# Linear-attention and mixture kernel on one core: order of the products' squares, places of the last chunk, and a weight load in three earlier quarters

## Chip, cores and metric

One core of one Trainium2 chip (trn2). The metric is the device time of one execution in microseconds; a change is told against the median of the runs of the kernel before, 618.05 us (617.24 to 618.30, 3 runs).

## What is computed

Inputs are q, k, v, a_re and a_im of 4 batches, 8 heads, 768 steps and 48 channels. The reference, cut to what matters:

```python
mag = sqrt(a_re**2 + a_im**2); scale = minimum(mag, 0.999) / (mag + 1e-6)
for t in range(768):                       # a complex decaying state for each head, 48 x 48
    S_re, S_im = ar*S_re - ai*S_im + k[t] v[t]^T, ar*S_im + ai*S_re
    y[t] = q[t] @ S_re
x = y as [3072, 384]
logits = x @ phi                           # 32 slots: 8 experts x 4
slot_in = softmax(logits, axis=tokens).T @ x
slot_out[e] = relu(slot_in[e] @ w1[e]) @ w2[e]      # w1[e] 384x1024, w2[e] 1024x384
x = softmax(logits, axis=slots) @ slot_out
out = relu(x @ w_in)**2 @ w_out            # 384 -> 2048 -> 384
```

## The kernel before, in words

Every engine has one program, written out by hand, and they meet only at semaphores. The recurrence is worked in 24 chunks (NT) of 128 steps, six (NC) to each of four batches (B). A batch p needs a **preparation** before its chunks: ScalarE (ACT) and VectorE (DVE) form the magnitudes of a in three tiles t (squares `take_squares`, sum `norm2`, logarithm and exponential `log_m2`, `magnitude`, `log_mag`, reciprocal `inv_mag`, L401, and the cut at 0.999 `bend`, L406); DVE multiplies (`normalise`, L767, three instructions); ACT makes the signed planes (`sign_planes`, L441, nine short copies). Then DVE runs the **chain of products** (`one`, L930): `init_products` (L777), 15 `product_step`s, three `block_step`s, the sum of squares of the first three quarters `square_sums(p, 0)` (L829, 128x1728), the turn factors (L835) and the last quarter's sum `square_sums(p, 1)` (128x576). The squares for these sums come from ACT (`product_squares`, L412: part 0 waits for the second-last block step, part 1 for the last). ACT takes the logarithm of the sums (`all_log_sums`, L428, two loads of the activation table around it), exponentials of it for the first chunk and then for the other five (`exponential`, L435).

The loops of DVE (L969) and ACT (L538) go over p and the chunk c: beside the chunks of batch p - 1 (n = 6(p - 1) + c) they prepare batch p (the chain) and batch p + 1 (the magnitudes). In this text "boundary p" is the place where loop p ends and loop p + 1 begins; boundaries 0, 1 and 2 are the ones with p < B - 1. On DVE a chunk is `key_query` (L878) twice with `weigh` (L870) between, `build_turn` (L896), and two masks `apply_mask` (L908) of the chunk before; steps of the chain stand between them as the shares of `parts` (L926) and `go` (L952) say. At c = 5 the order is: chunk's own work, chain up to the last block step, first sum of squares (for p > 0), the two masks, turn factors, second sum of squares; then the next p begins with the three `normalise`, `key_query`, `weigh` (which waits for the first exponential), `key_query`, `build_turn`, `init_products` (which waits for all signed planes).

On ACT at c = 4 the order is: three `inv_mag`, three `bend` (L555), then the chunk's copies of PE's results (`exponentials` of the softmax, `copy_kt` twice), the first squares (L591), `copy_y`, `copy_state`, the second squares, `copy_sums`, `copy_x`, `copy_raw`; at c = 5 `all_log_sums`, the first exponential, the signed planes, the other exponential, and only then `copy_y`.

TensorE (PE) does for each chunk `scores` (L1115, waits for the stacked inputs, which SyncE's DMAs bring over from DVE's output), `outputs` (L1152), `next_state` (L1131), a transpose of x (`turn_x`, L1188) and the `logits` (L1174); for every pair of chunks `flip` (L1199, transposes of the exponentials) and `weighted_sums` (L1210). `keep_busy` (L1110) fills gaps with idle matmuls. y has PSUM bank 5, x bank 6, the logits and the state share bank 4, scores use banks 0 to 3, the sums bank 7. Behind the last chunk come the slots' experts (PE L1287, L1309) and the last two products, from about 392 us on, which are half of the kernel's time.

The expert weights (16 tiles of 1.5 MB, two halves each from ACT's queue at the chunks' starts in loops 3 and 4, the others from SyncE's) go where the recurrence's tiles lie, as these come free. `EARLY` names six tiles that lie on the start of `big`. Three quarters of tile 6 lie on its columns 4 PF to 5 PF, which the recurrence never uses, and the last quarter on `N_` (5 PF), which the chain does use.

Of the kernel before, what the change touches and what calls it, by code (L numbers as in the profile page):

```python
# [42 lines left out]
def program(nc, a_all, xq_all, v_all, phi, w1, w2, w_in, w_out, out):  # L43
    with ExitStack() as ctx:
# [120 lines left out]
        def sk_ps(half, off, cols):  # L165
# [11 lines left out]
        et_ps = [ps[:, 6, NU * XR:NU * XR + 2 * SL]] * (NT - 1) + [ps[:, 4, 0:2 * SL]]  # L177
        sums_ps = ps[0:SR, 7, 0:DX]

# [6 lines left out]
        log_ready, inv_ready, bent, own_bent, an_ready = (sem("log_ready"), sem("inv_ready"), sem("bent"), sem("own_bent"),  # L186
                                                          sem("an_ready"))
# [6 lines left out]
        y_copied, x_done, x_copied = sem("y_copied"), sem("x_done"), sem("x_copied")  # L194
        lgt_done, raw_copied, max_ready = sem("lgt_done"), sem("raw_copied"), sem("max_ready")
# [32 lines left out]
        LOADED = [48 if k == 5 else 32 if k in EARLY + [10] else 16 for k in range(2 * NX)]  # L228
# [129 lines left out]
        def _(act):  # L358
# [82 lines left out]
            def sign_planes(b, t):  # L441
                act.wait_ge(an_ready, DT * b + t + 1)
# [23 lines left out]
            def copy_y(m):  # L466
                act.wait_ge(y_done, m + 1)
                if m >= 2:
                    act.wait_ge(x_done, m - 1)
                nc.scalar.activation(xts[:, m % 2], y_ps, ACT.Copy).then_inc(y_copied, 1)  # L470

            def copy_raw(m):
# [4 lines left out]
                nc.scalar.activation(eb[0:SR, j % 2, m % 2 * CH:(m % 2 + 1) * CH], lgt_ps, ACT.Copy, scale=-1.0).then_inc(raw_copied, 1)  # L477
# [60 lines left out]
            for p in range(B + 1):  # L538
                for c in range(NC + 2 * (p == B)):
                    n = (p - 1) * NC + c  # L540
                    if p == B - 1:
# [4 lines left out]
                    if p < B - 1:  # L546
# [7 lines left out]
                        elif c == 4:  # L554
                            for t in range(DT):  # L555
                                inv_mag(p + 1, t)
                            for t in range(DT):
                                bend(p + 1, t)
# [12 lines left out]
                    if p == B and c < NC:  # L571
# [3 lines left out]
                        load_half(NC + c)  # L575
# [15 lines left out]
                    if p < B and c == NC - 2:  # L591

                        product_squares(p, int(p == B - 1), 0)
                        product_squares(p, int(p == B - 1), 1)
# [15 lines left out]
                    if p < B - 1:  # L610
# [5 lines left out]
                        elif c == 4:  # L616
                            product_squares(p, 1, 0)
                            product_squares(p, 1, 1)
                    if pair is not None:
# [5 lines left out]
                    if n == NT:  # L625
                        copy_raw(n - 1)
# [841 lines left out]
```

## Time and profile before

| | |
|---|---|
| runs of the kernel before | 618.05 us median, 617.24 to 618.30 |
| the profiled execution | 617.78 us, span 616.1 us, mean granted clock of TensorE 0.934 |
| busy over the span | PE 512.4, DVE 392.4, ACT 339.4, POOL 138.4 us |
| up to about 60 us | DVE alone: magnitudes and the chain of batch 0 |
| 60 to 283 us | loops 1 to 3: chunks 0 to 17 beside the chains |
| 283 to 356 us | loop 4: chunks 18 to 23 |
| 356 to 392 us | experts |
| from 392 us | last products, PE busy throughout |

The views give, for one profiled execution, start and duration of instructions in microseconds from the span's first one; in brackets stands how long the engine had been idle and what ended that.

### The profile page before, as it was taken

The numbers are of one execution on the slowest core, as the hardware profiler recorded it, in microseconds if no ns is written. First come the engines' busy times: TensorE is split into PE (matmuls) and PEld (weight loads), VectorE is DVE, ScalarE is ACT, GpSimd is POOL, SyncE is SP. The second block draws the span as 40 slices with busy tenths as digits, with TensorE's granted clock in tenths as the row PEclk, the third lists the DMA queues.
The fourth block names the chain that finished last, engine by engine and source line by source line (L and its number), as shares of the span: only waits on it lengthen the run. The fifth ranks groups of instructions, "written<-read, shape, count | busy, mean of one in ns | idle before, by whom it ended". The sixth has DMA issues, their size and how long they took to land.

```text
span 616.1 us, 11719 instructions
## 1 busy us (share of the span) xinstructions
PE 512.4 (83%) x4566; PEld 386.4 (63%) x4566; DVE 392.4 (64%) x649; ACT 339.4 (55%) x593; POOL 138.4 (22%) x118
## 2 busy tenths in 40 slices
PE   1000459995998869997999999999999999999997
PEld 1000147774667646775788644578888888888886
DVE  5899999979999799995353151599423333233322
ACT  6818714697456953375243412676655555555653
POOL 7000000000000000000000000266555555555553
PEclk9655589997999979997999999999999999999999
DMA  7400575647655358886799999200101001010101
GB/s 272 153 1 0 113 207 129 146 93 193 170 119 147 71 152 205 231 210 145 190 278 257 422 426 421 99 1 2 53 0 53 0 1 51 2 51 2 53 0 52
DMA packets 41319, 79.59 MB, mean 129 GB/s; under 512 B 7344, under 2 KB 28976, under 8 KB 40112
## 3 DMA queue, kind: packets, MB, share of 16 engines
q1 hardware_dynamic: 39104, 67.44, 38.3%
q10 hardware_dynamic: 2160, 11.40, 5.3%
q8 instruction: 36, 0.59, 0.4%
q14 instruction: 19, 0.16, 0.1%
HBM read 55.12 MB, written 4.72 MB: 97 GB/s over the span
## 4 chain that ended last, share of the span: by engine, by line
PE 61%; DVE 24%; ACT 5%; issue 5%; DMA 3%; SPq 2%; DVEq 0%; ACTq 0%
PE ps L1397 10%; PE ps L1393 10%; PE ps L1394 10%; PE ps L1127 7%; PE ps L1113 4%; DVE tt L798 4%; PE ps L1367 3%; DVE big L772 3%; DVE tt L800 3%; DVE big L804 3%; PE ps L1184 2%; PE ps L1170 2%; DMA stk<-xout 2%; PE ps L1167 2%; PE ps L1287 2%
## 5 line engine op out<-in xcount | busy, mean ns | idle before, releaser
L1092 DVE TENSOR_TENSOR qs<-rs 128x512 f32<-128x512 f32 x96 | 82.7, 861 | 118.8 <-ACT rs L674 118.8
L735 POOL TENSOR_TENSOR hlo<-qs,hhi 128x512 fp32r<-128x512 f32 x96 | 126.1, 1313 | 125.0 <-DVE qs L1092 119.8
L1113 PE MATMUL ps<-ident 128*32 128x512 bf16 x274 | 81.3, 408 | 52.7 <-DVE xout L894 52.7
L1393 PE MATMUL ps<-hhi,who 128*128 128x512 f32 x285 | 110.9, 389 | 0.0
L1394 PE MATMUL ps<-hhi,wlo 128*128 128x512 f32 x285 | 110.9, 389 | 0.0
L674 ACT ACTIVATE rs<-ps 128x512 f32<-128x512 f32 x96 | 57.4, 598 | 82.2 <-PE ps L1367 82.1
L1127 PE MATMUL ps<-stk 112*128 112x224 f32 (+1 forms) x384 | 77.8, 358 | 12.7 <-DMA stk<-xout 12.7
L1127 PEld LDWEIGHTS ps<-stk 112*128 112x128 f32 x384 | 69.5, 199 | 23.9 <-DMA stk<-xout 18.3
L1397 PE MATMUL ps<-hlo,who 128*128 128x512 f32 x285 | 80.5, 391 | 0.1
L727 POOL MEMSET sinz<- 128x768 f32 x1 | 0.7, 738 | 335.9 <-PE ps L1170 335.9
L1113 PEld LDWEIGHTS ps<-ident 128*32 128x32 bf16 x274 | 23.0, 100 | 77.7 <-DVE xout L894 53.0
L678 ACT ACTIVATE hhi<-rs 128x512 fp32r<-128x512 f32 x96 | 60.8, 633 | 3.1
L1397 PEld LDWEIGHTS ps<-hlo,who 128*128 128x128 f32 x285 | 53.2, 188 | 12.2 <-POOL hlo L735 1.3
L1393 PEld LDWEIGHTS ps<-hhi,who 128*128 128x128 f32 x285 | 53.5, 188 | 11.2
L1394 PEld LDWEIGHTS ps<-hhi,wlo 128*128 128x128 f32 x285 | 53.5, 188 | 11.1
L915 DVE TENSOR_TENSOR asb<-ps,mask 128x512 f32<-128x512 f32 x48 | 32.5, 686 | 28.7 <-ACT kts L458 14.5
L458 ACT ACTIVATE kts<-ps 128x384 f32<-128x384 f32 x40 | 19.5, 487 | 52.4 <-PE ps L1127 52.4
L894 DVE TENSOR_TENSOR xout<-big,xq 128x768 f32<-128x768 f32 x48 | 45.7, 953 | 0.5
L1367 PE MATMUL ps<-cst,ust 128*128 128x512 f32 x96 | 37.4, 392 | 0.2 <-DVE ust L1074 0.2
L1170 PE MATMUL ps<-asb,vr 128*48 128x128 f32 x384 | 35.5, 273 | 0.0
L1167 PE MATMUL ps<-stk,st 112*48 112x128 f32 x320 | 31.8, 276 | 0.0
L1184 PE MATMUL ps<-xts,phs 112*32 112x128 f32 x576 | 28.3, 294 | 3.4 <-issue 2.9
(152 smaller groups left out, 795.5 us busy)
## 6 DMA issues: line engine op xcount, KB each, us to landing
stk<-xout SPq DMA_DIRECT2D x144, 128.0 KB, 3.7
wt<-in_w SPq DMA_DIRECT2D x8, 1536.0 KB, 15.2
wt<-in_w ACTq DMA_DIRECT2D x14, 768.0 KB, 6.1
big<-in_a_all SPq DMA_DIRECT2D x12, 768.0 KB, 5.5
xq<-in_xq SPq DMA_DIRECT2D x24, 384.0 KB, 4.2
vr<-in_v_all SPq DMA_DIRECT2D x24, 192.0 KB, 4.1
out<-ost SPq DMA_DIRECT2D x5, 768.0 KB, 3.5
wins<-in_w_in SPq DMA_DIRECT2D x1, 3072.0 KB, 19.8
```

The source lines that it names most:

```text
L674: nc.scalar.activation(rs[:, i % NQS, :], ps[:, i % 2, :], ACT.Relu).then_inc(relu_ready, 1)
L678: nc.scalar.activation(hhi[:, i % NHS, :], rs[:, i % NQS, :], ACT.Square).then_inc(hi_ready, 1)
L735: pool.tensor_tensor(hlo[:, i % NHS, :], qs[:, i % NQS, :], hhi[:, i % NHS, :].bitcast(F32), ALU.subtract).then_inc(lo_ready, 1)
L894: dve.tensor_tensor(o, e, x, ALU.mult).then_inc(kq_ready, 1)
L1092: dve.tensor_tensor(qs[:, i % NQS, :], rs[:, i % NQS, :], rs[:, i % NQS, :], ALU.mult).then_inc(sq_ready, 1)
L1113: nc.tensor.matmul(ps[P - SL:P, bank, :], idb[:, 0:SL], idle, start=True, stop=True)
L1127: last = nc.tensor.matmul(ps[:, h // 2, h % 2 * SK:h % 2 * SK + cols], x[:, 0:CH], x[:, CH:CH + cols], start=True, stop=True)
L1170: last = nc.tensor.matmul(y, vr[:, n % NV, h * D:(h + 1) * D], asb[:, n % 2, h], start=(c == 0), stop=True)
L1367: nc.tensor.matmul(ps[:, i % 2, :], ust[:, f * P:(f + 1) * P], cst[:, t * TW:(t + 1) * TW], start=True, stop=True).then_inc(g_done, 1)
L1393: nc.tensor.matmul(accs[k], wh[k], hi, start=(f == 0), stop=False)
L1394: nc.tensor.matmul(accs[k], wl[k], hi, start=False, stop=False)
L1397: last = nc.tensor.matmul(accs[k], wh[k], lo, start=False, stop=(f == F2B - 1))
```

## The change

Five things are done, all by hand in the engines' programs.

- **Squares and masks (loops 0 to 2).** On ACT `product_squares(p, 0, ...)` goes to the top of c = 4, in the place of `inv_mag` and `bend`; these go behind `copy_state` of c = 4, with the second squares between them. On DVE `square_sums(p, 0)` no longer stands ahead of the last masks but behind them (p < 3).
- **Batch 0's last plane.** The last `normalise` is split in two, imaginary part first with a semaphore of its own.
- **The last chunk.** y, logits and x of chunk 23 get PSUM banks 0, 1 and 2, and flip 22 bank 3. PE runs outputs(22), outputs(23), flip(21), logits(22), logits(23), weighted_sums(10), turn_x(22), turn_x(23). Half of the last y, the last two x and the sums of pair 10 are copied by DVE.
- **Weight tile 6.** Three quarters are loaded at c = 1, 3, 5 of loop 2, the last quarter at c = 0 of loop 4, instead of two halves at c = 0 and c = 1 of loop 4.

```diff
@@ -174,8 +174,12 @@
         lgt_ps = ps[0:SR, 4, DM:DM + CH]
-        et_ps = [ps[:, 6, NU * XR:NU * XR + 2 * SL]] * (NT - 1) + [ps[:, 4, 0:2 * SL]]
+        et_ps = [ps[:, 6, NU * XR:NU * XR + 2 * SL]] * (NT - 2) + [ps[:, 3, 0:2 * SL], ps[:, 4, 0:2 * SL]]
         sums_ps = ps[0:SR, 7, 0:DX]
+        last_y = ps[:, 0, :].rearrange("p (u t) -> p u t", u=NU)
+        last_lgt = ps[0:SR, 1, 0:CH]
+        last_x = ps[:, 2, 0:NU * XR].rearrange("p (u r) -> p u r", u=NU)
@@ -183,8 +187,8 @@
         squares, own_squares, m2_ready, m2_log, mag_ready = sem("squares"), sem("own_squares"), sem("m2_ready"), sem("m2_log"), sem("mag_ready")
-        log_ready, inv_ready, bent, own_bent, an_ready = (sem("log_ready"), sem("inv_ready"), sem("bent"), sem("own_bent"),
-                                                          sem("an_ready"))
+        log_ready, inv_ready, bent, own_bent, im_ready, an_ready = (sem("log_ready"), sem("inv_ready"), sem("bent"),
+                                                                    sem("own_bent"), sem("im_ready"), sem("an_ready"))
         m_squares, m_log, m_ready, signed = sem("m_squares"), sem("m_log"), sem("m_ready"), sem("signed")
@@ -192,6 +196,7 @@
         y_copied, x_done, x_copied = sem("y_copied"), sem("x_done"), sem("x_copied")
+        last_y_copied = sem("last_y_copied")
         lgt_done, raw_copied, max_ready = sem("lgt_done"), sem("raw_copied"), sem("max_ready")
@@ -225,7 +230,7 @@
-        LOADED = [48 if k == 5 else 32 if k in EARLY + [10] else 16 for k in range(2 * NX)]
+        LOADED = [64 if k == 6 else 48 if k == 5 else 32 if k in EARLY + [10] else 16 for k in range(2 * NX)]
         ld_w = [sem(f"ld_w{k}") for k in range(2 * NX)]
@@ -439,7 +444,10 @@
             def sign_planes(b, t):
-                act.wait_ge(an_ready, DT * b + t + 1)
+                if b == 0 and t == DT - 1:
+                    act.wait_ge(im_ready, 1)
+                else:
+                    act.wait_ge(an_ready, DT * b + t + 1)
                 if b and t == 0:
@@ -467,6 +475,10 @@
                     act.wait_ge(x_done, m - 1)
+                if m == NT - 1:
+                    nc.scalar.activation(xts[0:D, m % 2], last_y[0:D], ACT.Copy).then_inc(last_y_copied, 1)
+                    return
                 nc.scalar.activation(xts[:, m % 2], y_ps, ACT.Copy).then_inc(y_copied, 1)
@@ -474,7 +486,8 @@
                     act.wait_ge(flipped, 2 * j - 2)
-                nc.scalar.activation(eb[0:SR, j % 2, m % 2 * CH:(m % 2 + 1) * CH], lgt_ps, ACT.Copy, scale=-1.0).then_inc(raw_copied, 1)
+                nc.scalar.activation(eb[0:SR, j % 2, m % 2 * CH:(m % 2 + 1) * CH], last_lgt if m == NT - 1 else lgt_ps, ACT.Copy,
+                                     scale=-1.0).then_inc(raw_copied, 1)
@@ -538,6 +551,9 @@
                     n = (p - 1) * NC + c
+                    if p == B - 2 and c % 2:
+                        load_part(6, c // 2, c // 2 + 1)
                     if p == B - 1:
@@ -552,10 +568,8 @@
                         elif c == 4:
-                            for t in range(DT):
-                                inv_mag(p + 1, t)
-                            for t in range(DT):
-                                bend(p + 1, t)
+                            product_squares(p, 0, 0)
+                            product_squares(p, 0, 1)
                     if p == B - 1 and c == NC - 2:
@@ -572,7 +586,10 @@
                             act.wait_ge(kq_ready, 2 * NC * (B - 1))
-                        load_half(NC + c)
+                        if c == 0:
+                            load_part(6, 3, 4)
+                        if c >= 2:
+                            load_half(NC + c)
@@ -588,10 +605,10 @@
                             log_mag(p + 1, 1)
-                    if p < B and c == NC - 2:
-                        product_squares(p, int(p == B - 1), 0)
-                        product_squares(p, int(p == B - 1), 1)
+                    if p == B - 1 and c == NC - 2:
+                        product_squares(p, 1, 0)
+                        product_squares(p, 1, 1)
                     if c == NC - 1 and p < B - 1:
@@ -614,19 +631,22 @@
                         elif c == 4:
+                            for t in range(DT):
+                                inv_mag(p + 1, t)
                             product_squares(p, 1, 0)
                             product_squares(p, 1, 1)
-                    if pair is not None:
+                            for t in range(DT):
+                                bend(p + 1, t)
+                    if pair is not None and n != NT - 1:
                         copy_sums(pair)
...
                         copy_y(n)
-                    if n == NT:
-                        copy_raw(n - 1)
+                    if 1 <= n < NT - 1:
+                        copy_x(n - 1)
                     if 1 <= n <= NT:
-                        copy_x(n - 1)
-                    if 1 <= n < NT:
                         copy_raw(n - 1)
@@ -769,6 +789,13 @@
                     dve.wait_ge(bent, DT * (b - 1) + t + 2 if b else 1)
+                if b == 0 and t == DT - 1:
+                    for c, done in ((1, im_ready), (0, an_ready)):
+                        dve.scalar_tensor_tensor(out=grid(PL[0] + c * PF + t * PT, [1, PT]), in0=grid(U_ + t * PT, [1, PT]),
+                                                 scalar=KNEE, in1=grid(RAW + c * PF + t * PT, [1, PT]), op0=ALU.subtract,
+                                                 op1=ALU.mult, reverse0=True).then_inc(done, 1)
+                    return
                 dve.scalar_tensor_tensor(out=grid(PL[b % 2] + t * PT, [PF, 2], [1, PT]),
@@ -993,7 +1020,7 @@
                         go(p, mid)
-                    if 0 < p < B and c == NC - 1:
+                    if p == B - 1 and c == NC - 1:
@@ -1015,7 +1042,29 @@
                         norm2(p + 1, 2)
+            def last_copy_y():
+                dve.wait_ge(y_done, NT)
+                dve.wait_ge(x_done, NT - 2)
+                dve.tensor_copy(xts[R1:R1 + D, (NT - 1) % 2], last_y[R1:R1 + D]).then_inc(last_y_copied, 1)
+            def last_copy_x(m):
+                dve.wait_ge(x_done, m + 1)
+                dve.wait_ge(sums_done, (m - NX3) // 2 + 1)
+                x = (last_x if m == NT - 1 else x_ps)[:, 0]
+                x = bass.AP(ps, x.offset, [list(x.ap[0]), [XR, NU], [R1, 2], [1, D]])
+                dve.tensor_copy(xsb[:, m % NX3, 0:DM].rearrange("p (u r e) -> p u r e", u=NU, r=2), x).then_inc(x_copied, 1)
+            def last_copy_sums(j):
+                dve.wait_ge(sums_done, j + 1)
+                dve.tensor_copy(sums[0:SR, :], sums_ps).then_inc(sums_copied, 1)
+            last_copy_y()
             running_max(NT // 2 - 1)
+            last_copy_sums(NT // 2 - 2)
+            for m in (NT - 2, NT - 1):
+                last_copy_x(m)
@@ -1151,7 +1200,7 @@
                 b, c = divmod(n, NC)
-                if n:
+                if 0 < n < NT - 1:
                     pe.wait_ge(y_copied, n)
@@ -1162,7 +1211,7 @@
                             h = 2 * u + r
-                            y = y_ps[R1 * r:R1 * r + D, u, :]
+                            y = (last_y if n == NT - 1 else y_ps)[R1 * r:R1 * r + D, u, :]
                             if part == 0:
@@ -1173,34 +1222,47 @@
-                pe.wait_ge(y_copied, m + 1)
+                if m == NT - 1:
+                    pe.wait_ge(last_y_copied, 2)
+                else:
+                    pe.wait_ge(y_copied, m + 1)
                 pe.wait_ge(s_copied, turns(min(m + 2, NT)))
-                if m:
+                if m == NT - 1:
+                    pe.wait_ge(masked, 2 * NT)
+                elif m:
                     pe.wait_ge(raw_copied, m)
...
                     for g in range(0, SR, SL):
-                        last = nc.tensor.matmul(lgt_ps[g:g + SL], phs[0:XR, u, :], xts[0:XR, m % 2, u, :], start=(u == 0),
+                        last = nc.tensor.matmul((last_lgt if m == NT - 1 else lgt_ps)[g:g + SL], phs[0:XR, u, :], xts[0:XR, m % 2, u, :], start=(u == 0),
                                                 stop=(u == NU - 1))
...
-                pe.wait_ge(y_copied, m + 1)
-                if m:
+                if m == NT - 1:
+                    pe.wait_ge(last_y_copied, 2)
+                else:
+                    pe.wait_ge(y_copied, m + 1)
+                if m == NT - 1:
+                    pe.wait_ge(masked, 2 * NT)
+                elif m:
                     pe.wait_ge(x_copied, m)
...
                 for u in range(NU):
-                    last = nc.tensor.transpose(x_ps[:, u, :], xts[0:XR, m % 2, u, :], ident[0:XR, 0:XR])
+                    last = nc.tensor.transpose((last_x if m == NT - 1 else x_ps)[:, u, :], xts[0:XR, m % 2, u, :], ident[0:XR, 0:XR])
                 last.then_inc(x_done, 1)
...
                 pe.wait_ge(exp_done, m // 2 + 1)
-                pe.wait_ge(x_copied, m // 2 * 2 + (2 if m >= NT - 4 else 3))
-                if m == NT - 1:
+                if m < NT - 2:
+                    pe.wait_ge(x_copied, m // 2 * 2 + (2 if m >= NT - 4 else 3))
+                if m == NT - 2:
+                    pe.wait_ge(masked, 2 * NT)
+                elif m == NT - 1:
                     pe.wait_ge(raw_copied, NT)
@@ -1239,22 +1301,24 @@
                     outputs(n - 1)
+                if n == NT - 1:
+                    outputs(n)
                 if pair is not None:
...
                     next_state(n)
+                if n == NT - 1:
+                    logits(n - 1)
+                    logits(n)
                 if pair is not None:
...
                     weighted_sums(pair)
-                if n == NT - 1:
-                    outputs(n)
-                if n == NT:
-                    logits(n - 1)
                 if 1 <= n <= NT:
...
                     turn_x(n - 1)
-                if 1 <= n < NT:
+                if 1 <= n < NT - 1:
                     logits(n - 1)
```

## Rows read from the trace of the kernel before

**Rows 1.** DVE's timeline, boundary 1: start, duration, what; in brackets idle before.

```profile
121.23 0.24 DVE L811 COPY pexp<-big 128x144 f32<-128x144 f32 x1
...
131.47 1.96 DVE L833 TENSOR_TENSOR big<-big 128x1728 f32<-128x1728 f32 x1 [3.66 <-ACT big L420]
...
136.50 5.08 DVE L772 SCALAR_TENSOR_TENSOR big<-big 128x1536 f32<-128x1536 f32 x3
...
144.70 0.18 DVE L782 COPY a<-big 128x36 f32<-128x36 f32 x1
```

**Rows 2.** Timelines at boundary 2: DVE, PE, ACT, DVE.

```profile
205.40 1.96 DVE L833 TENSOR_TENSOR big<-big 128x1728 f32<-128x1728 f32 x1 [4.08 <-ACT big L420]
...
200.97 0.27 PE L1207 MATMUL ps<-ident,eb 64*128 64x64 f32 x1 [1.08 <-ACT eb L491]
...
208.74 1.28 ACT L430 ACT_TABLE_LOAD   x1
...
218.64 0.18 DVE L782 COPY a<-big 128x36 f32<-128x36 f32 x1
```

**Rows 3.** Busy table: window, length, PE, PEld, DVE, ACT, POOL busy, PEclk, DMA share, GB/s.

```profile
340.81:355.89 15.08, 13.06 (x163) 9.18 (x160) 2.22 (x4) 6.43 (x19) 0.74 (x1) 1.00 1.03 426
122.51:134.93 12.42, 11.35 (x163) 8.46 (x161) 8.70 (x14) 12.13 (x22) 0.00 (x0) 1.00 0.53 112
```

**Rows 4.** Chain of waits where the experts' weights are first read.

```profile
358.16 5.37 PE ps L1287 x46
```

**Rows 5.** ACT's timeline at boundary 1.

```profile
122.51 2.30 ACT L404 ACTIVATE big<-big 128x768 f32<-128x768 f32 x3
...
128.26 3.18 ACT L420 ACTIVATE big<-big 128x1728 f32<-128x1728 f32 x2
...
132.31 0.49 ACT L464 ACTIVATE st<-ps 112x384 f32<-112x384 f32 x1 [0.27 <-PE ps L1148]
...
132.70 1.25 ACT L420 ACTIVATE big<-big 128x576 f32<-128x576 f32 x2
...
134.93 1.28 ACT L430 ACT_TABLE_LOAD   x1
...
140.21 0.51 ACT L448 ACTIVATE big<-big 128x384 f32<-128x384 f32 x1
...
144.35 1.81 ACT L439 ACTIVATE big<-big 128x1920 f32<-128x1920 f32 x1
```

**Rows 6.** PE's timeline at the same place.

```profile
127.46 0.27 PE L1207 MATMUL ps<-ident,eb 64*128 64x64 f32 x1 [1.07 <-ACT eb L491]
...
146.68 1.01 PE L1196 MATMUL ps<-ident,xts 112*128 112x112 f32 x4 [6.50 <-ACT xts L470]
```

**Rows 7.** ACT's timeline behind a weight issue at c = 4 of loop 3.

```profile
268.04 3.18 ACT L420 ACTIVATE big<-big 128x1728 f32<-128x1728 f32 x2 [0.17 <-issue]
```

**Rows 8.** Timelines of ACT (first two) and DVE at boundary 0.

```profile
55.07 3.18 ACT L420 ACTIVATE big<-big 128x1728 f32<-128x1728 f32 x2 [0.40 <-DVE big L827]
...
60.75 1.28 ACT L430 ACT_TABLE_LOAD   x1
...
71.39 0.18 DVE L782 COPY a<-big 128x36 f32<-128x36 f32 x1
```

**Rows 9.** ACT's timeline, last signed plane of batch 0.

```profile
21.73 0.52 ACT L448 ACTIVATE big<-big 128x384 f32<-128x384 f32 x1 [0.16 <-DVE big L772]
```

**Rows 10.** PE's timeline, last chunk: its three stops.

```profile
351.15 0.75 PE L1184 MATMUL ps<-xts,phs 112*32 112x128 f32 x15 [0.48 <-ACT eb L477]
...
353.73 0.34 PE L1207 MATMUL ps<-ident,eb 64*128 64x64 f32 x2 [0.97 <-ACT eb L491]
...
355.89 0.85 PE L1264 MATMUL ps<-sel,sums 96*128 96x32 f32 x6 [0.58 <-ACT sums L511]
```

**Rows 11.** DMA issues of the stacked inputs, loop 2, then loop 3: KB, us to landing.

```profile
stk<-xout SPq DMA_DIRECT2D x36, 128.0 KB, 3.5
...
stk<-xout SPq DMA_DIRECT2D x36, 128.0 KB, 3.6
```

## The prediction

> **What bounds the kernel now.** I read the busy share in forty slices first (which engine is full where), then the timelines of the engines at the three boundaries and in the last chunk, then the chain of waits behind them. From 60 to 283 us DVE is the full engine. Its timeline there has two large holes, 3.66 us at 131.47 and 4.08 us at 205.40, both ahead of the first sum of squares and both ended by ACT's squares [rows 1, 2]. ACT is nearly full there: 12.13 of the 12.42 us from 122.51 to 134.93 are busy [rows 3]. So at a boundary ACT is the bound and DVE waits for it. From 340.81 to the experts PE is the bound, with 2.02 us of stops in 15.08 [rows 3]. The experts' weights bound nothing: the chain goes through PE's own matmuls there [rows 4].
>
> The profiled execution took 617.78 us, 0.27 under the median. The sum is made against it.
>
> **Boundary 1.** Before, ACT's order at c = 4 was: inverses 2.2 us from 122.51, bends as long, exponentials of the softmax and kt copies to 128.26, first squares 3.1, copies of y and of the state (132.31), second squares and three copies 2.2, table load at 134.93 [rows 5]. PE's results lay ready when ACT came to them.
>
> After, step by step:
> - The first squares run from 122.5 (the block step they wait for ended at 121.2 [rows 1]) to 125.6, the exponentials to 126.0. PE's flip had stood 1.07 us for these, until 127.46, so its scores ended at 126.4 [rows 6]; all that PE does behind the flip comes 1.06 us earlier.
> - The copies of y and state now stand ahead of inverses and bends, and wait for PE. The state's copy began at 132.31 behind a wait of 0.27 for PE [rows 5]; it now begins at 131.25 and ends at 131.65. ACT has its kt copies done at 127.0, so between there and 131.25 lie 4.2 us with 0.8 us of work: **3.4 us of new idle** on the engine that bounds the boundary.
> - Inverses to 133.85, second squares to 135.0, bends to 137.2, three copies to 138.3. The table load starts at 138.3 instead of 134.93.
>
> On DVE the hole of 3.66 us goes: the last block step ended at 127.8 (131.47 less 3.66), masks to 129.0, first sum to 130.9, turn factors to 132.2. But the second sum now waits for squares that end at 135.0: a new hole of 2.8. It ends at 135.7, and the three `normalise` start there instead of at 136.50 [rows 1], each bend just in time: 0.8 us gained. `weigh` then needs the first exponential, and the signed planes follow on ACT. The first plane began 5.28 us behind the table load and the last ended 4.14 later (140.21, 144.35) [rows 5]: now 143.6 and 147.75. `init_products` stood at 144.70 [rows 1], 0.35 behind the last plane, and now starts at 147.75: the next chain is **3.05 us later**. Up to the next boundary DVE has no wait but for PE, which itself waits for the stacked inputs that DVE sends, so I take all of it. Bounds: 0.8 gained, if ACT's late load cost nothing behind it, and 3.4 lost.
>
> **Boundary 2** has the same pattern. The flip is freed of 1.08 us at 200.97 [rows 2]; 4.8 us behind its start the state is done, as at boundary 1, now at 204.7. Then 0.4 + 2.2 + 1.15 + 2.2 + 1.1: table load at 211.8 instead of 208.74, last plane 9.4 later at 221.2, and `init_products` stood at 218.64 [rows 2]: +2.6. The third quarter of tile 6 is issued on ACT right ahead of the table load; behind such an issue ACT stood 0.17 us [rows 7]. Together **+2.75**, bounds as above.
>
> **Boundary 0** has no chunks, so ACT waits for no PE. But the first squares wait for the block step until 55.07 [rows 8], and inverses and bends, which had been done by then, now stand behind them. Squares to 58.2, inverses to 60.4, second squares to 61.55, bends to 63.75: there the table load, which was at 60.75. DVE's `normalise` at 63.2 finds its bends, `weigh` at 69.06 just finds the exponential, the signs end at 73.2, and `init_products` was at 71.39 [rows 8]: **+1.8**, bounds 0 and 3.0.
>
> The masks ahead of the sum let PE's last scores of a batch start earlier. That gives nothing: PE then stood 6.50 us until ACT copied y behind both exponentials [rows 6], and this copy comes 3.4 later. PE's own delay is not added, since it waits for stacked inputs in the chunks behind.
>
> **Batch 0's plane.** ACT's last signs had waited 0.16 us for DVE [rows 9]. The split frees them: **-0.15**. The extra instruction's overhead lies beside the signs; without them it would cost some 0.1.
>
> **The last chunk.** PE's three stops are 0.48, 0.97 and 0.58 [rows 10]. The first (logits of 23 behind the raw copy) goes with the second place for logits. The second (flip behind the exponential) goes too: both logits are done at about 349.3 and the exponential at 350.5, while PE does the sums of pair 10 and both transposes until 351.95. The third, the copy of the last sums, stays. A wait of about 0.2 inside weighted_sums(10) also goes. In exchange DVE copies the last x, 0.5 us, between the last transpose and the last sums, beside the flips and their copies, which take as long. 0.48 + 0.97 + 0.2 less 0.05 is **-1.6**. Bounds: 0, if DVE's copies come last, and -2.0, all stops.
>
> **Weight tile 6.** No wait for weights shows [rows 4], so an earlier landing gives 0. It could cost by contention with the stacked inputs. Loop 3 carries six halves of weights from ACT's queue and loop 2 none, and the stacked inputs landed in 3.6 and 3.5 us [rows 11]; three quarters are a quarter of that traffic, so 0. The issue that falls away at c = 1 of loop 4 saves nothing, as ACT is idle there.
>
> A rule speaks against this part. The Trainium skill (DMA: Bandwidth & Descriptors, "Issuing engines are not separate DMA queues") says that transfers started by different engines run on the same 16 DMA engines and interleave. By it a quarter in flight could hold a stacked input for as long as it runs itself; the two loops differ by 0.1 us only, so the trace bears little of that out.
>
> **Sum:** 1.8 + 3.05 + 2.75 - 0.15 - 1.6 = +5.85. 617.78 + 5.85 = 623.6, or 623.9 from the median; I say 623.7.
>
> **Rivals.**
> - *ACT's new order costs nothing behind the squares* (faster). Place: the table load at c = 5. If ACT's waits for y and the state do not open, or DVE does not wait for the signs, the holes of 3.66 and 4.08 close and nothing follows: 617.78 - 7.74 - 1.75 = 608.3. It decides as soon as the three boundaries cost less than 1.75 us together. For it: both holes are real. Against it: 0.35 us between the last plane and `init_products`, and an ACT that is full [rows 3]. Half-way, 0.8 gained at two boundaries and no loss, the time is 614.4. Together 0.14.
> - *The quarters collide with stacked inputs.* 393 KB at the 426 GB/s of full DMA engines [rows 3] are 0.92 us; three collisions in front of scores that PE waits for give +2.8, 626.4. This is the case in which the skill's rule would hold in full. 0.06.
> - *The last chunk gives nothing*, as DVE's copies end last: 625.2. 0.06.
> - *The new order is inert*, neither holes nor delays moved: only the last chunk's gain or nothing, 616 to 618. 0.04.
> - *The forecast*: 0.70, its own range 621.5 to 625.5.
>
> **Range and chances.** 619.5 to 626.5 holds the forecast, the collisions, a last chunk without gain, and boundaries at half of what I worked out. About 0.2% is what a measurement of this kernel can tell from no change. Faster: 0.14 and half of the inert case, 0.16. Same: 0.04, the other half and boundaries that just cancel the rest. Slower: what is left, 0.80.
>
> **What would show it.** Right: no hole ahead of DVE's first sum; at boundaries 1 and 2 holes of 2 to 3 us ahead of the second sum and of 1 to 2 ahead of `weigh` and of `init_products`; ACT idle 3.4 us at c = 4; the first table load near 63.6; `init_products` 1.6, 4.7 and 7.4 us later than before; from the last scores to the slots' first product 13.5 us instead of 15.1. Wrong: table loads where they were, or DVE without holes at the boundaries. A stacked input landing in over 4.5 us in loop 2 would show the collision.

## The result, and the profile after

The changed kernel took 623.17 us (median of 6 runs, 621.21 to 625.52) against 617.30 us (6 runs, 616.49 to 618.30): ratio 1.0094, interval 1.0070 to 1.0118, slower. The forecast was 623.7. Beside other kernels on another chip it took 620.81 us (10 runs) against 617.74 (29 runs): ratio 1.0048, interval 1.0020 to 1.0077, slower again, but by 3.1 us and not 5.9. The trace taken there shows the same boundaries (e10), so why the medians lie closer together there stays open. The profiled execution has a span of 621.5 us, 5.4 more than before.

`init_products` starts each chain, so its four starts cut the recurrence into stretches; the last scores and the slots' first product mark the last chunk. In microseconds, from the timelines of the two profiled executions:

| stretch | before | after | difference |
|---|---|---|---|
| start to chain 0 | 23.30 | 22.85 | -0.45 |
| chain 0 to chain 1 (boundary 0) | 48.09 | 50.02 | +1.93 |
| chain 1 to chain 2 (boundary 1) | 73.31 | 76.30 | +2.99 |
| chain 2 to chain 3 (boundary 2) | 73.94 | 78.19 | +4.25 |
| chain 3 to the last chunk's scores | 122.17 | 121.58 | -0.59 |
| the last chunk | 15.08 | 12.44 | -2.64 |
| the rest | 260.21 | 260.12 | -0.09 |

DVE's timeline after, at boundaries 0, 1 and 2 (in brackets how long it had stood, and for whom):

```profile
72.87 0.18 DVE L809 COPY a<-big 128x36 f32<-128x36 f32 x1 [1.71 <-ACT big L459]
...
136.54 0.76 DVE L860 TENSOR_TENSOR big<-big 128x576 f32<-128x576 f32 x1 [2.87 <-ACT big L425]
...
145.03 0.56 DVE L903 TENSOR_TENSOR xq<-xq,big 128x384 f32<-128x384 f32 x1 [1.80 <-ACT big L444]
...
149.17 0.18 DVE L809 COPY a<-big 128x36 f32<-128x36 f32 x1 [1.72 <-ACT big L459]
...
214.73 0.76 DVE L860 TENSOR_TENSOR big<-big 128x576 f32<-128x576 f32 x1 [2.87 <-ACT big L425]
...
227.36 0.18 DVE L809 COPY a<-big 128x36 f32<-128x36 f32 x1 [1.72 <-ACT big L459]
```

L809 is `init_products`, L860 of 128x576 the second sum, L903 `weigh`. The one hole of before [rows 1] is gone from the first sum, and three others stand in its place: 2.87, 1.80 and 1.72 us. All three wait for ACT, and boundary 2 has the same.

ACT's timeline after, at boundary 1:

```profile
124.03 3.17 ACT L425 ACTIVATE big<-big 128x1728 f32<-128x1728 f32 x2
...
130.36 0.60 ACT L482 ACTIVATE xts<-ps 128x512 f32<-128x512 f32 x1 [1.62 <-PE ps L1219]
...
132.68 0.49 ACT L472 ACTIVATE st<-ps 112x384 f32<-112x384 f32 x1 [1.60 <-PE ps L1197]
...
133.06 2.30 ACT L409 ACTIVATE big<-big 128x768 f32<-128x768 f32 x3
...
135.26 1.24 ACT L425 ACTIVATE big<-big 128x576 f32<-128x576 f32 x2
...
136.41 2.30 ACT L415 ACTIVATE big<-big 128x768 f32<-128x768 f32 x3
...
139.63 1.28 ACT L435 ACT_TABLE_LOAD   x1
...
144.90 0.51 ACT L456 ACTIVATE big<-big 128x384 f32<-128x384 f32 x1
...
149.04 1.80 ACT L444 ACTIVATE big<-big 128x1920 f32<-128x1920 f32 x1
```

The squares (L425) come first, at 124.03. Then ACT stands 1.62 us for the outputs and 1.60 us for the state, and only then come inverses (L409), second squares, bends (L415), copies, and the table load at 139.63. From the start of the work of c = 4 to the table load it was 12.42 us [rows 5], and now is 15.60. PE's timeline, where it waits for the copy of y behind both exponentials:

```profile
151.38 1.01 PE L1255 MATMUL ps<-ident,xts 112*128 112x112 f32 x4 [10.82 <-ACT xts L482]
```

This wait was 6.50 us [rows 6]. At boundary 0 ACT has no copies of PE's results, but the squares hold up inverses and bends:

```profile
54.59 3.18 ACT L425 ACTIVATE big<-big 128x1728 f32<-128x1728 f32 x2 [4.80 <-DVE big L854]
...
63.33 1.28 ACT L435 ACT_TABLE_LOAD   x1
```

The table load was at 60.75 [rows 8].

The last chunk: busy table of the stretch, then PE's timeline, then DVE's.

```profile
348.94:361.38 12.44, 11.78 (x164) 8.95 (x161) 4.49 (x8) 5.19 (x16) 0.74 (x1) 1.00 1.03 423
```

```profile
355.30 1.62 PE L1238 MATMUL ps<-xts,phs 112*32 112x128 f32 x39
...
359.21 0.34 PE L1269 MATMUL ps<-ident,eb 64*128 64x64 f32 x2
...
361.38 0.85 PE L1328 MATMUL ps<-sel,sums 96*128 96x32 f32 x6 [0.60 <-ACT sums L524]
```

```profile
359.32 0.56 DVE L1057 COPY xsb<-ps 128x384 f32<-128x384 f32 x1 [0.24 <-PE ps L1255]
```

Of 2.02 us of stops PE has 0.66 left, 0.60 of them ahead of the slots' product. The logits of both chunks run as one row of 39 matmuls and more (355.30), the flips follow the last transpose without a stop (359.21), and DVE's copy of the last x ends with ACT's copies of the flips (359.88 and 359.86).

### The profile page after: what moved, and what is told of

It reads as the page before. It is cut to its first block, busy times and chain, and to the rows that moved or that the text cites. A ratio compares the mean times of both kernels' runs of the same rounds, so it can differ in the third digit from the quotient of the medians.

```text
span 621.5 us, 11723 instructions
## 1 busy us (share of the span) xinstructions
PE 510.1 (82%) x4566; PEld 386.2 (62%) x4566; DVE 395.4 (64%) x654; ACT 338.1 (54%) x590; POOL 138.3 (22%) x118
## 4 chain that ended last, share of the span: by engine, by line
PE 67%; DVE 13%; ACT 10%; DMA 4%; issue 3%; SPq 2%; ACTq 0%; DVEq 0%
PE ps L1461 11%; PE ps L1457 10%; PE ps L1458 10%; PE ps L1176 9%; PE ps L1162 5%; PE ps L1431 4%; DVE tt L825 3%; DVE tt L827 3%; DVE big L831 3%; DMA big<-in_a_all 2%; PE ps L1219 2%; PE ps L1216 2%; PE ps L1238 2%; PE ps L1194 2%; PE ps L1351 2%
## 5 line engine op out<-in xcount | busy, mean ns | idle before, releaser
L1162 PEld LDWEIGHTS ps<-ident 128*32 128x32 bf16 x274 | 22.7, 99 | 76.8 <-DVE xout L921 52.7
L942 DVE TENSOR_TENSOR asb<-ps,mask 128x512 f32<-128x512 f32 x48 | 32.5, 685 | 29.8 <-ACT kts L466 14.8
L1255 PE MATMUL ps<-ident,xts 112*128 112x112 f32 x96 | 15.3, 284 | 24.6 <-ACT xts L482 24.6
L1255 PEld LDWEIGHTS ps<-ident,xts 112*128 112x128 f32 x96 | 9.9, 146 | 35.5 <-ACT xts L482 26.5
```

What stands on the lines that cost most here:

```text
L1162: nc.tensor.matmul(ps[P - SL:P, bank, :], idb[:, 0:SL], idle, start=True, stop=True)
```

## Experiments

All times are compared with runs of the kernel before on the same chip. Executions of one kernel on these chips differ by several microseconds (the last section says what part of that is), so one per mille is not resolved; the stretches between fixed marks in a profiled execution show more. These are the stretches of all kernels, one profiled execution of each, in microseconds:

| kernel | chain 0 to 1 | 1 to 2 | 2 to 3 | last chunk |
|---|---|---|---|---|
| before | 48.1 | 73.3 | 73.9 | 15.1 |
| after | 50.0 | 76.3 | 78.2 | 12.4 |
| e1, last chunk alone | 48.1 | 73.8 | 73.8 | 12.4 |
| e2, both orders alone | 50.0 | 76.8 | 76.8 | 15.7 |
| e3, quarters alone | 48.1 | 73.5 | 73.7 | 15.1 |
| e4, DVE's order alone | 48.1 | 73.9 | 73.7 | 15.1 |
| e5, after without quarters | 50.0 | 76.1 | 76.6 | 12.4 |
| e6, ACT's order alone | 50.0 | 75.8 | 76.6 | 15.1 |
| e7, after, quarters at c = 3, 4, 5 | 50.0 | 75.5 | 76.5 | 12.4 |
| e8, interleaved order | 48.1 | 72.1 | 73.1 | 15.7 |
| e9, the gains together | 48.1 | 73.2 | 73.4 | 12.4 |
| e10, after once more | 50.0 | 76.3 | 78.6 | 12.4 |
| e11, after with ACT's order of before | 48.1 | 73.1 | 73.9 | 12.4 |

In e2 and e8 the granted clock was 0.50 in the last 2 us of the last chunk (1.00 throughout it before), which is why they show 15.7.

Marks nearer to a boundary show its cost with less from elsewhere in it. From DVE's first `key_query` of c = 5 to the next `init_products`, boundaries 1 and 2 took 23.31 and 23.75 us before. In all six traces with ACT's order of the change (after, e2, e5, e6, e7, e10) they took 26.3 to 26.4, in e4 and e11, with DVE's order alone, 23.1 and 23.4 to 23.5, and in e8 and e9 22.8 and 23.1. So ACT's order costs 3.0 and 2.5 us there. What the table shows beside that arises earlier: in the scores of chunk 1 (last section), and in loop 2 with the quarter of c = 1.

**Theory: order.** The loss is ACT's order at c = 4, which puts waits for PE ahead of work that DVE waits for. **Rivals:** the quarters of tile 6 collide with other transfers; or DVE's order (the sum behind the masks) is what costs.

**e1, the last chunk alone.**

```diff
+ last_y, last_lgt, last_x in banks 0, 1, 2, flip 22 in bank 3, PE's order and the copies of chunk 23 as in the change
```

> The last chunk's part alone, put into the kernel before. Theory (the order of ACT's work costs, the last chunk gains): 2.6 us faster than the kernel before, since the stretch from the last scores to the slots' first product took 15.08 us before and 12.44 after; chunks 0 to 22 stay as they are. Rival (the last chunk gains nothing by itself and the shorter stretch came from another state of the clock or from weights that had landed earlier): within 0.5 us of the kernel before.

616.04 us against 618.68, ratio 0.9969 (0.9948 to 0.9991): 0.1 to 0.5% faster, and its last chunk takes 12.44 us as in the whole change. The gain is the part's own.

**e2, both orders alone**, and **e6, ACT's order alone.**

```diff
 # ACT, c = 4 of loops 0 to 2 (e2 and e6)
+product_squares(p, 0, 0); product_squares(p, 0, 1)
 # exponentials, kt, y, state: copies of PE's results
-bend and inv_mag ahead of them
+inv_mag x3, product_squares(p, 1, .) x2, bend x3 behind copy_state
 # DVE (e2 only)
-if 0 < p < B and c == NC - 1:
+if p == B - 1 and c == NC - 1:
     one(p)
```

> The two reorderings alone (first squares ahead of inverses and bends on ACT, first sum behind the masks on DVE) in the kernel before. Theory (order): 7 to 8 us slower, namely 1.9 at boundary 0, 3.0 at boundary 1 and 2.7 at boundary 2, with holes of 2.9, 1.8 and 1.7 us on DVE ahead of the second sum, weigh and init_products. Rival (the weight quarters in batch three are what costs, the order nothing): within 1 us of the kernel before.

> The kernel before with ACT's new order alone; DVE still takes the first sum ahead of the masks. Theory (what costs is ACT's waits for y and the state in front of inverses and bends): boundaries as with both reorderings, init_products 50.0, 76.8 and 76.8 us apart, 7 to 8 us slower than the kernel before; at boundaries 1 and 2 PE's last scores start 1.9 us later than with both, and nothing follows from that. Rival (the harm comes from the sum behind the masks): within 2 us of the kernel before.

e2 took 625.11 us against 618.68, ratio 1.0121 (1.0079 to 1.0164). e6 took 626.29 against 618.41, ratio 1.0134 (1.0100 to 1.0169). ACT's order alone makes the whole loss of the boundaries, and DVE's order adds nothing to it: from c = 5 on, both boundaries take 26.27 us in e2 and in e6. DVE's timeline of e6 at boundary 1:

```profile
136.43 0.76 DVE L835 TENSOR_TENSOR big<-big 128x576 f32<-128x576 f32 x1 [2.87 <-ACT big L420]
...
144.92 0.56 DVE L878 TENSOR_TENSOR xq<-xq,big 128x384 f32<-128x384 f32 x1 [1.80 <-ACT big L439]
...
149.06 0.18 DVE L784 COPY a<-big 128x36 f32<-128x36 f32 x1 [1.72 <-ACT big L451]
```

These are the changed kernel's three holes to 0.01 us, with the first sum still ahead of the masks. One expectation fell: PE's last scores of the batch did not start later in e6 than in e2 (both 13.4 us ahead of the next `init_products`). PE comes to them only then, so the order of masks and sum does not reach PE.

**e4, DVE's order alone.**

```diff
-if 0 < p < B and c == NC - 1:
+if p == B - 1 and c == NC - 1:
     one(p)
```

> DVE's order alone in the kernel before: masks ahead of the first sum of squares, ACT untouched. Theory: the masks (1.28 us) run inside the hole ahead of the first sum at boundaries 1 and 2, whose end is set by ACT, so the first sum starts at the same time and what follows it comes 1.2 us earlier at each, if ACT lets it: normalise has its bends, but init_products stood only 0.35 behind the last signed plane, so 0.3 to 0.4 us each and 0.6 to 0.8 us faster in all. Rival (the sum behind the masks is the harmful part): 2 us or more slower.

615.85 us against 618.68, ratio 0.9972 (0.9941 to 1.0003): not told from no change, and no loss. DVE's timeline:

```profile
132.06 1.96 DVE L833 TENSOR_TENSOR big<-big 128x1728 f32<-128x1728 f32 x1 [2.32 <-ACT big L420]
...
145.06 0.18 DVE L782 COPY a<-big 128x36 f32<-128x36 f32 x1 [0.88 <-ACT big L451]
```

The hole of 3.66 us is 2.32, since the masks lie in it, and the rest comes back as 0.88 ahead of `init_products`, whose start ACT's signs set. From the first `key_query` of c = 5 to `init_products` this is 0.2 and 0.3 us less than before at the two boundaries. The rival that the sum behind the masks costs is out.

**e3, the quarters alone.**

```diff
+if p == B - 2 and c % 2:
+    load_part(6, c // 2, c // 2 + 1)
 # loop 4, c = 0 and 1
-load_half(6), load_half(7)
+load_part(6, 3, 4) at c = 0
```

> Only the three quarters of weight tile 6 in loop 2 (and the last quarter in loop 4) in the kernel before. Theory: up to 1.5 us slower, because the quarter at c = 1 is in flight with the raw tile of batch three, which then lands later; ACT waits for it, copies y late, and PE stops. Rival (quarters are the whole loss): 4 us or more slower. Second rival (no cost): within 0.3 us.

617.85 us against 618.68, ratio 0.9980 (0.9949 to 1.0010): no change that can be told. ACT's timeline at c = 1 of loop 2 (ACTq is its DMA queue):

```profile
160.77 2.22 ACTq L372 DMA_DIRECT2D wt<-in_w  x1
...
167.34 0.84 ACT L381 ACTIVATE big<-big 128x768 f32<-128x768 f32 x1 [0.53 <-DMA big<-in_a_all]
```

The issue took 2.22 us, but the raw tile was there at 167.3, and ACT had stood for it only 0.53 us. The delay that was expected of this run did not come. So the first rival is out as the main cause. Yet in the changed kernel loop 2 was 1.3 us longer than boundary 2 explains, which the next three runs take up.

**e5, the change without quarters**, **e7, with later quarters**, and **e10, the change once more.** ACT's timeline of the changed kernel at c = 1 of loop 2, PE's, and its DMA issues there:

```profile
165.04 1.89 ACTq L377 DMA_DIRECT2D wt<-in_w  x1
...
174.98 0.84 ACT L386 ACTIVATE big<-big 128x768 f32<-128x768 f32 x1 [4.08 <-DMA big<-in_a_all]
```

```profile
177.10 0.60 PE L1255 MATMUL ps<-ident,xts 112*128 112x112 f32 x4 [2.75 <-ACT xts L482]
```

```profile
big<-in_a_all SPq DMA_DIRECT2D x1, 768.0 KB, 9.2
```

The raw tile of batch 3, issued 0.7 us behind the quarter, needed 9.2 us. ACT stood 4.08 us for it, so it copied y late, and PE stood 2.75 us.

```diff
 # e5: change without its hunks for tile 6
 # e7: change with
-if p == B - 2 and c % 2:
-    load_part(6, c // 2, c // 2 + 1)
+if p == B - 2 and c >= 3:
+    load_part(6, c - 3, c - 2)
```

> The changed kernel with weight tile 6 loaded as before (two halves in loop 4, no quarters in loop 2). In the trace of the changed kernel the raw tile issued 0.7 us behind the quarter of c = 1 landed after 9.2 us, ACT waited 4.08 us for it and PE 2.75 us for the copy of y behind it. Theory (the quarter at c = 1 is what delays that tile): these two waits shrink to the 0.7 us and 0 of before, the third init_products follows the second by 76.8 us instead of 78.2, and the time falls by 1.4 us. Rival (the new order alone moves the tile's load into other transfers): the waits stay, and so does the time.

> The changed kernel with its three quarters issued at c = 3, 4 and 5 of loop 2 instead of 1, 3 and 5, behind the last raw tile's landing. Theory: as without quarters, init_products 76.8 us apart in loop 2, PE's stop of 2.75 us gone, 1.4 us faster than the changed kernel; a quarter at c = 4 or 5 delays ACT's busy stretch by at most 0.3 us. Rival (any quarter in loop 2 costs): 78 us apart.

> The changed kernel once more, beside the others on one chip. Theory: as on record, 0.9% slower than the kernel before; init_products 50.0, 76.3 and 78.2 us apart, with PE's stop of 2.75 us in loop 2 if the quarter's collision with the raw tile is a matter of the program's order. Rival (it was a matter of one execution): 76.6 us in loop 2 and no such stop.

ACT's timeline of e5 at the same place, and its DMA issue of the tile:

```profile
171.08 0.84 ACT L386 ACTIVATE big<-big 128x768 f32<-128x768 f32 x1 [0.46 <-DMA big<-in_a_all]
```

```profile
big<-in_a_all SPq DMA_DIRECT2D x1, 768.0 KB, 5.9
```

Without the quarter the tile lands in 5.9 us, ACT stands 0.46, and PE's stop for y is gone. In e7 ACT stood 0.30 us, and PE's stop was gone too. The stretch is 76.6 and 76.5 us. e10 repeats the collision: 78.6 us, ACT 4.36, PE 3.02. So both traces of this program have the collision, and they are 1.6 to 2.2 us longer in loop 2 than e5 and e7. In e3 the tile was issued first, 0.05 us ahead of the quarter (160.72 and 160.77), and landed in 6.6 us, as before (6.5); there the quarter was the slow one, with 9.0.

A part of this cost goes through TensorE's clock. Behind its stops of 2.75 and 3.02 us PE had a granted clock of 0.50 from 179.2 to 181.2 us in both traces, and took 7.3 us from the transpose of x to the end of the next scores. In e11 (below), with a stop of 2.25 us, the clock stayed at 1.00 and the same work took 5.7. Why it fell in the two and not in e11 wasn't tried.

In time e5 is 621.42 against 618.41 (ratio 1.0060, 1.0038 to 1.0083), e7 622.00 (1.0072, 1.0046 to 1.0097), e10 620.81 against 617.74 (1.0048, 1.0020 to 1.0077): these intervals overlap. By the medians e5, without the collision, lies as far above the kernel before (3.0 us) as e10 with it (3.1), so only the traces tell the kernels apart.

**e11, ACT's order put back in the changed kernel.**

```diff
 # ACT at c = 4 as before; last chunk, split, DVE's order and quarters as in the change
```

> The changed kernel with only ACT's order at c = 4 put back to that of before; DVE's order, the last chunk, the split and the quarters stay. Theory: the 7.6 us of the boundaries go, the gains of the last chunk and the start stay, 3 us faster than the kernel before (within 1 us, by what the quarters do). Rival (the sum behind the masks costs too): slower than the kernel before.

614.08 us against 617.74, ratio 0.9932 (0.9907 to 0.9957). Undoing this one part turns 0.5% slower on this chip (e10; 0.9% on the first) into 0.7% faster. But the collision is here too, with ACT's order of before: the tile was issued 0.46 us behind the quarter and landed in 9.0 us. ACT's and PE's timelines:

```profile
169.32 0.84 ACT L386 ACTIVATE big<-big 128x768 f32<-128x768 f32 x1 [3.58 <-DMA big<-in_a_all]
```

```profile
171.44 0.60 PE L1253 MATMUL ps<-ident,xts 112*128 112x112 f32 x4 [2.25 <-ACT xts L482]
```

ACT stood 3.58 us and PE 2.25, and yet loop 2 took 73.9 us, as before: PE's next scores came 29.8 us behind `init_products`, where they lie in e3 as well, and DVE was not held up. In the changed kernel they came at 31.1, and in e10 at 32.2. So the late tile does not need the new order: in the three traces that have it the tile was issued behind the quarter, and in e3, which has not, ahead of it. It cost time only in the two traces where PE stood longer and the clock fell behind the stop.

**e8, an order that keeps both**, and **e9, it and the other gains.** The first squares do belong first; inverses and bends fit in ACT's waits for PE.

```diff
 # ACT, c = 4 of loops 1 and 2; loop 0 as before
+product_squares(p, 0, 0); product_squares(p, 0, 1)
 exponentials, copy_kt, copy_flipped, copy_kt
+inv_mag x3
 copy_y, copy_flipped
+bend x3
 copy_state
 product_squares(p, 1, 0); product_squares(p, 1, 1)
 # DVE as in e4; e9 adds the last chunk and the split of batch 0
```

> The kernel before with DVE's new order and a third order for ACT at boundaries 1 and 2: first squares, exponentials and kt copies, inverses, copy of y, bends, copy of the state, second squares; boundary 0 as before. Theory: inverses and bends now lie in ACT's waits for PE (127.0 to 131.25), so the table load comes at about 134.2 instead of 134.9 and the last signed plane 0.7 us earlier; DVE has a hole of about 0.9 ahead of the second sum and 1.5 ahead of init_products, which starts 1.0 us earlier at each of the two boundaries: 2 us faster than the kernel before. Rival (first squares in front of the others cost whatever the rest): 4 us slower or more.

> The kernel before with the last chunk's part, batch 0's split normalise, the masks ahead of the first sum, and the interleaved order of ACT at boundaries 1 and 2 (boundary 0 and weight tile 6 as before). Theory: the gains are at different places and add up: 0.3 at the start, 2 to 2.5 at the two boundaries and 2.6 in the last chunk, 5 us faster than the kernel before. Rival (behind the last chunk something else is late, or PE runs at a lower granted clock after it): no more than the 2 us of the last chunk alone.

ACT's and DVE's timelines of e8 at boundary 1:

```profile
121.56 3.17 ACT L420 ACTIVATE big<-big 128x1728 f32<-128x1728 f32 x2
...
133.72 1.28 ACT L430 ACT_TABLE_LOAD   x1
```

```profile
132.83 0.76 DVE L843 TENSOR_TENSOR big<-big 128x576 f32<-128x576 f32 x1 [1.62 <-ACT big L420]
...
143.27 0.18 DVE L792 COPY a<-big 128x36 f32<-128x36 f32 x1 [1.48 <-ACT big L451]
```

From ACT's start on c = 4 to `init_products` it is 21.7 us (121.56 to 143.27), against 22.2 before (122.51 to 144.70) and 25.1 after (124.03 to 149.17); at boundary 2 21.9 against 22.6. The order itself gives 1.2 us, not the 2 expected; what e8's table row shows beyond that comes from chunk 1 (last section). In time e8 can't be told from before: 617.82 against 618.41, ratio 0.9989 (0.9962 to 1.0016). e9 took 614.65 against 617.74, ratio 0.9928 (0.9901 to 0.9954). It beats both kernels, and e11 does as well; between the two nothing can be told. It was expected to be 5 us faster than before and is 3.1. One stop of e9's trace is new. PE's timeline in the experts' stage, and the DMA issue of tile 14, taken from a window that holds it alone (357.3 to 357.6):

```profile
370.49 1.04 PE L1383 MATMUL ps<-ident,c 128*128 128x128 f32 x8
373.05 2.78 PE L1353 MATMUL ps<-wt,sinz 128*32 128x512 f32 x24 [1.52 <-issue]
```

```profile
wt<-in_w SPq DMA_DIRECT2D x1, 1536.0 KB, 15.6
```

The tile lands at some 372.9, and the products that need it, of `hidden(3)`, start at 373.05, 1.5 us late. In e11 the tile took 13.7 us and was there just in time; in the changed kernel 14.0, and before 11.4. e1, e5 and e9 have the short last chunk without the quarters, and behind `transpose_c` these products start 0.3, 0.2 and 1.6 us later than in the kernels that have both (after, e7, e10, e11). Only e5 differs from its partner (after) in the quarters alone; for e1 and e9 the quarters as the cause are not shown.

## Why the prediction was right

- **Boundary 1.** Forecast +3.05, measured +2.99 (2.96 from c = 5 on). The table load came 3.2 us later in ACT's work (15.60 less 12.42) where 3.4 was forecast, and DVE's holes were 2.87, 1.80 and 1.72 where 2.8 and twice 1 to 2 were forecast. e6 shows that ACT's order alone makes them.
- **Boundary 0.** Forecast +1.8, measured +1.93, by the mechanism told: squares ahead of inverses and bends.
- **Boundary 2.** Forecast +2.75, measured +4.25 in the stretch. The boundary itself gave what was forecast: e5 and e7 have 76.6 and 76.5 us, 2.7 and 2.6 more than before (2.5 from c = 5 on). The other 1.6 us come with the quarter at c = 1: a raw tile that landed late, PE's stop behind it, and a granted clock of 0.50 behind the stop. The step that failed is "three quarters are a quarter of that traffic, so 0". It looked at the stacked inputs alone, which indeed landed in 3.5 us as before, and not at the raw tile that ACT waits for. The rival of the collision put the price (0.9 us for each of three) on the wrong transfer: one quarter of three collided, with another victim. The rule of the Trainium skill (DMA: Bandwidth & Descriptors, "Issuing engines are not separate DMA queues"), that transfers started by different engines run on the same 16 DMA engines and interleave, agrees with this trace: the tile took 9.2 us against 5.9 without the quarter (e5), and the quarter 8.5 us against 3.2 and 3.4 for the two later ones.
- **Weight tile 6.** Forecast 0 for the earlier landing. That holds beside the long last chunk (e3). Beside the short one the weights are what comes last at `hidden(3)`, and the quarters are worth 0.2 us there (e5 against the changed kernel): a term that was not seen, as the chain of before showed no wait for a weight [rows 4]. In e9 the same products were 1.6 us late; whether the quarters would have spared it that wasn't tried.
- **Batch 0's plane.** Forecast -0.15. DVE's wait ahead of the first chain fell from 1.61 to 1.28 us, 0.33. The stretch to chain 0 became 0.45 shorter, since the first loads landed 0.1 to 0.2 us earlier in this execution, while the extra instruction took back 0.06 (1.82 us for the two against 1.76 for one).
- **The last chunk.** Forecast -1.6, measured -2.64 in the changed kernel, and the same in e1. The mechanism is the one told (the stops of 0.48 and 0.97 gone, 0.58 left), the size was short by 1.0 us. The term that was mis-sized is "a wait of about 0.2 inside weighted_sums(10)". Before, PE stood there for the copy of the flip, which its weight loads show:

```profile
346.09 0.14 PEld L1220 LDWEIGHTS ps<-xsb,lgx 128*32 128x32 f32 x2 [0.53 <-ACT lgx L507]
```

From these sums' start to PE's next work it was 1.44 us (345.41 to 346.85), and now 0.76 (357.07 to 357.83): 0.7 gained and not 0.2. Another 0.5 us, which the forecast didn't have, came where matmuls of one kind now stand in one row: 0.3 at the logits, 0.15 at the outputs, less than 0.1 at the last transpose.

- **The sum** came out right, +5.85 forecast and +5.4 in the trace, in part by luck: an unseen 1.6 us of loss and an unseen 1.0 us of gain nearly cancel. PE also did the logits of chunk 17 at a higher granted clock this time (0.50 before from 280.7 to 283.4, 0.78 after from 289.9 to 292.4), which is about 0.7 us of gain.
- **The faster rival** fell at the place named for it: the waits for y and the state did open (1.62 and 1.60 us), and DVE did wait for the signs.

## What to carry to other kernels

When a hole on the full engine is ended by another engine that is itself full, moving the awaited work to the front pays only if what is moved back doesn't land behind a wait for a third engine: count the idle time that the new order opens, not only the one that it closes. Put work with no input from a slow partner into the waits for that partner, as e8 does. A transfer that is moved earlier is to be checked against every transfer in flight there that some engine waits for, not against the most frequent one alone, and so is the granted clock behind a stop that it makes. And where DMAs are full for the stage that follows, shortening the work ahead of it brings the weights into the chain: the two parts are to be judged together.

## What the runs showed that I had not expected

**A DMA issue on ACT's queue can take 2 us.** The quarter's issue at c = 1 took 1.89 to 2.37 us in all four traces that have it (after, e10, e3, e11); SyncE was issuing the next inputs or the 768 KB tile at that moment. Those at c = 3, 4 and 5 took 0.33 to 0.38. ACT's next instruction waits for it. That SyncE issues at the moment isn't enough by itself: e7's issue at 211.04 us took 0.33 with SyncE at small ones. What makes it long wasn't tried.

**The same work takes different times by where TensorE's clock rises.** The scores of chunk 1 follow a pause of PE of 4 to 8 us. PE's timelines of e8 and e9:

```profile
89.86 4.97 PE L1137 MATMUL ps<-stk 112*128 112x224 f32 x16 [6.07 <-DMA stk<-xout]
```

```profile
89.39 6.24 PE L1178 MATMUL ps<-stk 112*128 112x224 f32 x16 [4.29 <-DMA stk<-xout]
```

Both are the same 16 matmuls; at the full clock they take 3.29. The granted clock was 0.50 from 88 to 92 us and 0.68 from 92 to 94 in e8, and 0.50 from 90 to 94 and 0.65 from 94 to 96 in e9. DVE waits for them later, which moved chain 2 by up to 1.4 us from kernel to kernel (e7 and e2). The experts show it too: the granted clock is 1.00 in the executions of before and after, and at half (1.2 GHz of 2.4) for part of that stage in e2, e4, e6, e8 and e10. Busy tables of before and of e2:

```profile
355.00:360.00 5.00, 4.42 (x39) 2.64 (x38) 2.62 (x5) 0.72 (x2) 0.29 (x1) 1.00 1.01 428
360.00:365.00 5.00, 5.00 (x49) 2.22 (x45) 3.18 (x6) 1.80 (x3) 0.00 (x0) 1.00 1.00 419
```

```profile
360.00:365.00 5.00, 3.58 (x19) 2.17 (x19) 0.11 (x1) 2.00 (x7) 0.00 (x0) 0.60 1.01 426
365.00:370.00 5.00, 5.00 (x27) 2.70 (x31) 3.37 (x6) 0.84 (x1) 0.29 (x1) 0.50 1.02 433
```

The stretch from the slots' first product to the end was 260.1 to 260.5 us with the clock full (261.8 in e9, with its wait for tile 14), and 261.8 to 263.8 where it fell; after and e10 are one program, at 260.1 and 261.8. So a fallen clock is part of what makes executions of one kernel differ by several microseconds here. Why it falls in one execution and not in another wasn't tried.
